# The first expert's weights fetched and split within the last feed-forward group

## The reference

```python
    logits = x @ w_gate
    e_idx = np.argmax(logits, axis=1)
    probs = softmax(logits); gate_w = probs[np.arange(N), e_idx]
    eom = 1.0 / (1.0 + np.exp(-(x @ w_output_gate)))
    for e in range(E):
        mask = e_idx == e
        h = np.maximum(x[mask] @ w1[e], 0.0)          # 512 -> 1024
        ye = h @ w2[e]                                # 1024 -> 512
        out[mask] = gate_w[mask, None] * eom[mask, e, None] * ye
```

## Time and profile before

| | us |
|---|---|
| runs of the kernel | 1080.41, 1082.92, 1083.64 (median 1082.92) |
| profiled execution | 1083.53, of which the span is 1081.2 |
| PE busy in the span | 1051.2 (97%) |
| DVE, ACT, POOL busy | 411.1, 293.1, 123.2 |

### The profile page before, as it was taken

One profiled execution on the slowest core, in us unless ns is written; L12 is line 12 of the kernel. 1 busy time (PEld: TensorE's weight loads), 2 busy tenths in 40 slices (PEclk: granted clock), 3 DMA queues, 4 the chain that ended last, 5 costly groups with the idle time before them and its releaser, 6 DMA issues.

```text
span 1081.2 us, 18273 instructions
## 1 busy us (share of the span) xinstructions
PE 1051.2 (97%) x6499; PEld 939.7 (87%) x6500; DVE 411.1 (38%) x794; ACT 293.1 (27%) x550; POOL 123.2 (11%) x113
## 2 busy tenths in 40 slices
PE   6989999999999999999999999998999999999997
PEld 5888999999999999999999999976788888888886
DVE  3454432323223223223222322458446444364542
ACT  2544332112112122121121121131334333243431
POOL 4770000000000000000000000023111211112111
PEclk9999999999999999999999999996999999999999
DMA  9996701001001001010010000060553533335311
GB/s 363 367 328 198 211 1 60 1 1 59 1 1 59 1 25 35 1 56 3 1 59 1 1 30 1 1 205 10 205 191 117 204 121 116 113 117 204 118 34 35
DMA packets 34090, 98.69 MB, mean 91 GB/s; under 512 B 4397, under 2 KB 10797, under 8 KB 34032
## 3 DMA queue, kind: packets, MB, share of 16 engines
q1 hardware_dynamic: 28976, 83.17, 22.5%
q0 software_dynamic: 4480, 13.90, 3.7%
q10 hardware_dynamic: 576, 0.79, 0.2%
HBM read 80.54 MB, written 18.09 MB: 91 GB/s over the span
## 4 chain that ended last, share of the span: by engine, by line
PE 93%; DMA 3%; DVE 3%; issue 0%; ACT 0%; POOL 0%; ACTq 0%; POOLq 0%; DVEq 0%
PE bank L941 37%; PE bank L959 18%; PE bank L1325 14%; PE bank L1301 13%; PE bank L1309 2%; PE bank L578 2%; DMA rows<-in_steps 2%; PE bank L529 1%; PE bank L630 1%; PE bank L543 1%; PE bank L564 1%; DMA qdec_t<-in_consts 1%; PE bank L744 1%; PE bank L753 1%; PE bank L1020 0%
## 5 line engine op out<-in xcount | busy, mean ns | idle before, releaser
L941 PE MATMUL bank<-x_hi,wab_hi 128*128 128x384 f32 x768 | 258.2, 336 | 0.0
L941 PE MATMUL bank<-x_hi,wab_lo 128*128 128x384 f32 x768 | 257.8, 336 | 0.0
L941 PE MATMUL bank<-x_lo,wab_hi 128*128 128x384 f32 x768 | 257.2, 335 | 0.0
L887 DVE TENSOR_TENSOR g_sb<-bank,b_sb 128x384 f32<-128x384 f32 x96 | 53.5, 557 | 370.9 <-PE bank L941 370.9
L941 PEld LDWEIGHTS bank<-x_hi,wab_hi 128*128 128x128 f32 x768 | 144.2, 188 | 4.2 <-issue 0.6
L941 PEld LDWEIGHTS bank<-x_lo,wab_hi 128*128 128x128 f32 x768 | 144.2, 188 | 3.6
L941 PEld LDWEIGHTS bank<-x_hi,wab_lo 128*128 128x128 f32 x768 | 144.1, 188 | 0.0
L705 ACT COPY b_sb<-bank 128x384 f32<-128x384 f32 x96 | 46.3, 482 | 257.3 <-PE bank L941 257.3
L959 PE MATMUL bank<-wo_hi,g_hi 128*128 128x512 f32 x288 | 115.7, 402 | 0.0
L959 PE MATMUL bank<-wo_hi,g_lo 128*128 128x512 f32 x288 | 113.4, 394 | 0.0
L959 PE MATMUL bank<-wo_lo,g_hi 128*128 128x512 f32 x288 | 113.2, 393 | 0.0
(11 more groups left out here) (161 smaller groups left out, 1201.0 us busy)
## 6 DMA issues: line engine op xcount, KB each, us to landing
raw<-in_w SPq DMA_DIRECT2D x64, 512.0 KB, 6.7
rows<-in_steps SPq DMA_DIRECT2D x20, 768.0 KB, 7.5
rows<-in_steps SPq DMA_DIRECT2D x24, 256.0 KB, 6.6
wab_raw<-in_weights SPq DMA_DIRECT2D x24, 256.0 KB, 7.2
x_dram<-y_sb SPq DMA_DIRECT2D x8, 768.0 KB, 4.1
xT_dram<-x_all SPq DMA_DIRECT2D x6, 768.0 KB, 12.1
x_raw<-xT_dram SPq DMA_DIRECT2D x6, 768.0 KB, 5.2
wo_raw<-in_weights SPq DMA_DIRECT2D x4, 768.0 KB, 9.7
```

The costliest lines, as they stand in the source:

```text
L887: nc.vector.tensor_tensor(g_sb[:, f % 2], bank[2 * (f % 2)][:, 0:GT], b_sb[:, f % 2], ALU.mult).then_inc(g_done, 1)
L941: ins = nc.tensor.matmul(bank[to][:, 0:GT], wab(w, f, j), x[s][:, k, :], start=(k == 0 and m == 0), stop=(k == KD - 1 and m == 2))
```

## The change

- **SP** loads w1 of expert 0 in the last group, two parts after step f=1 and two after f=3, and w2 likewise after f=5 and f=7, as the feed-forward weights under them fall free.
- **ACT** casts w1 after f=5 and f=6, three parts of w2 after the last step and the fourth behind the copies of y. **DVE** subtracts w1 after f=8, 9 and 10, and all of w2 in `dve_route`. **POOL** subtracts nothing any more.
- So that w1's two halves fit beside what is still in use, w1_hi and w1_lo share one buffer.
- **PE** transposes tile 1 into bank 3 directly behind the group, runs up(0) and puts the transposes of y and the logits between its matmuls; the last group's logits are made in strips as those of the other groups are (`pe_partial`, `pe_logits`). The sort stands within down(1), which is ahead of x_T(2) and up(2).
- POOL gathers tiles 2 and 3 together.

```diff
-    w1_hi = place("w1_hi", (P, 2 * KD * FE), F32R)
-    w1_lo = place("w1_lo", (P, 2 * KD * FE), F32R)
+    w1 = place("w1", (P, 2 * W1_SPAN), F32R)
+    w1_hi, w1_lo = w1[:, 0:W1_SPAN + KD * FE], w1[:, KD * FE:]
...
+    AT_W1_HI = {5: (0, 1), 6: (2, 3)}
+    AT_W1_LO = {AT_SCALE: (0, 1), AT_RANK: (2,), AT_FIRST: (3,)}
...
-                sp.wait_ge(a_done, GROUPS * KF)
-                load_expert(sp, raw1, w1_in, 0, raw1_in)
+                for half in range(2):
+                    sp.wait_ge(a_done, g * KF + 2 * half + 2)
+                    load_expert(sp, raw1, w1_in, 0, raw1_in, (2 * half, 2 * half + 1))
+                for half in range(2):
+                    sp.wait_ge(a_done, g * KF + 2 * half + 6)
+                    load_expert(sp, raw2, w2_in, 0, raw2_in, (2 * half, 2 * half + 1))
...
-        load_expert(sp, raw2, w2_in, 0, raw2_in)
...
+                if last and f in AT_W1_HI:
+                    split_w1(act, True, 0, AT_W1_HI[f])
...
-                split_w1(act, True, 0, (0,))
+                split_w2(act, True, 0, (0, 1, 2))
...
+                    if f in AT_W1_LO:
+                        split_w1(dve, False, 0, AT_W1_LO[f])
...
-        for t in range(TG):
-            pe.wait_ge(yT_read, TG * LAST + t + 1)
-            if t == 0:
-                pe.wait_ge(g_done, GROUPS * KF + 2)
-            for k in range(KD):
-                ins = nc.tensor.matmul(bank[3][:, t * 2 * NE:(t + 1) * 2 * NE], yT3[:, t, k, :], gates[:, k, :],
-                                       start=(k == 0), stop=(k == KD - 1))
-            ins.then_inc(logit_done, 1)
...
-        split_w1(dve, False, 0, (0,))
+        split_w2(dve, False, 0, (0, 1))
+        split_xe(dve, 1, 1)
...
-        split_w1(dve, False, 0, (1, 2))
-        dve.wait_ge(logit_done, TG * GROUPS)
-        v.tensor_copy(L3.rearrange("p t e -> p (t e)"), bank[3][:, 0:TG * 2 * NE]).then_inc(logit_read, TG)
+        split_w2(dve, False, 0, (2,))
+        dve_partial(dve, LAST, part_last)
+        split_w2(dve, False, 0, (3,))
+        dve_logits(dve, LAST)
...
-        split_xe(dve, 1, 1)
+        hT_rest(dve, 0)
...
-        hT_rest(dve, 0)
-
-        dve.wait_ge(w2_first_done, PARTS)
+        hT_rest(dve, 1)
...
-        split_w1(act, True, 0, (1, 2, 3))
+        split_w2(act, True, 0, (3,))
+        relu(0, True)
         act_exp(act, LAST)
         act_exp_og(act, LAST)
-        split_w2(act, True, 0, (0,))
-        relu(0, True, (0,))
-        split_w2(act, True, 0, (1,))
-        relu(0, True, (1,))
-        split_w2(act, True, 0, (2, 3))
...
-        part = slice((PARTS - 1) * PW, PARTS * PW)
-        pool.wait_ge(w1_hi_done, PARTS)
-        nc.gpsimd.tensor_tensor(w1_lo[:, part], raw1[:, part], w1_hi[:, part].bitcast(F32),
-                                ALU.subtract).then_inc(w1_first_done, 1)
-        for q in range(PARTS):
-            part = slice(q * PW, (q + 1) * PW)
-            pool.wait_ge(w2_hi_done, q + 1)
-            nc.gpsimd.tensor_tensor(w2_lo[:, part], raw2[:, part], w2_hi[:, part].bitcast(F32),
-                                    ALU.subtract).then_inc(w2_first_done, 1)
...
         gather(2)
+        gather(3)
...
-        pe_last_logits(pe)
-        up(0, 0, 0, {(0, 2): lambda: x_T(pe, 1, 1, 0, bank[4]), (1, 0): lambda: pe_counts(pe)})
-        pe.wait_ge(logit_read, TG * GROUPS + 1)
-        pe.wait_ge(h_read, 1)
-        up(1, 1, 0, {(1, 0): lambda: h_T(0)})
-        pe_sort(pe)
-        down(0, 0, None)
+        pe.wait_ge(g_done, GROUPS * KF + 2)
+        x_T(pe, 1, 1, 0, bank[3])
+        up(0, 0, 0, {(1, 0): lambda: pe_last_yT(pe), (1, 2): lambda: pe_partial(pe, LAST, yT_last)})
+        pe_logits(pe, LAST, part_last)
+        pe.wait_ge(h_read, 2)
+        up(1, 1, 0, {(1, 0): lambda: h_T(0), (1, 1): lambda: pe_counts(pe)})
+        down(0, 0, 0)
+        h_T(1)
+        down(1, 1, 0, {2: lambda: pe_sort(pe)})
         x_T(pe, 2, 0, 1, bank[4])
-        h_T(1)
...
         up(2, 0, run_of(run_even))
         x_T(pe, 3, 1, 1, bank[4])
-        down(1, 1, None)
         in_pairs(pe, pairs, pair)
```

More of the change, by code:

```diff
@@ L41 @@
 PW = KD * FE // PARTS
+W1_SPAN, W2_SPAN = 2 * KD * FE, KE * DM
 C_IDENT = 0
@@ L220, in build @@
     xe_lo = place("xe_lo", (P, 2, KD, P), F32R, where=x_raw_at + KD * GT * 4)
-    yT3 = place("yT3", (P, TG, KD, P), where=x_raw_at)
+    yT_last = place("yT_last", (P, KD, GT), where=x_raw_at)
     at[0] = x_raw_at
@@ L230, in build @@
     assert at[0] <= x_raw_at + KD * GT * 4
+    part_last = place("part_last", (P, GT), where=common)
     at[0] = common
@@ L634, in split_xe @@
         dve.wait_ge(xe_T_done, i + 1)
-        psum = bank[7 if isinstance(i, int) and i == 0 else 4].rearrange("p (k t) -> p k t", k=KD)
+        at_bank = {0: 7, 1: 3}.get(i, 4) if isinstance(i, int) else 4
+        psum = bank[at_bank].rearrange("p (k t) -> p k t", k=KD)
         nc.vector.tensor_copy(xe_hi[:, s], psum).then_inc(xe_done, 1)
@@ L638, in split_xe, with split_weight @@
         nc.vector.tensor_tensor(xe_lo[:, s], psum, xe_hi[:, s].bitcast(F32), ALU.subtract).then_inc(xe_done, 1)
-    def split_weight(eng, hi, run, raw, raw_in, w_hi_, w_lo_, hi_done, lo_done, parts):
+    def split_weight(eng, hi, run, raw, raw_in, w_hi_, w_lo_, span, hi_done, lo_done, parts):
         for q in parts:
-            to = bass.ds((run % 2) * (PARTS * PW) + q * PW, PW)
+            to = bass.ds((run % 2) * span + q * PW, PW)
             frm = raw[:, q * PW:(q + 1) * PW]
@@ L652, in split_w1 @@
     def split_w1(eng, hi, run, parts=range(PARTS)):
-        split_weight(eng, hi, run, raw1, raw1_in, w1_hi, w1_lo, w1_hi_done, w1_lo_done, parts)
+        split_weight(eng, hi, run, raw1, raw1_in, w1_hi, w1_lo, W1_SPAN, w1_hi_done, w1_lo_done, parts)
     def split_w2(eng, hi, run, parts=range(PARTS)):
-        split_weight(eng, hi, run, raw2, raw2_in, w2_hi, w2_lo, w2_hi_done, w2_lo_done, parts)
+        split_weight(eng, hi, run, raw2, raw2_in, w2_hi, w2_lo, W2_SPAN, w2_hi_done, w2_lo_done, parts)
     def in_groups(eng, group):
@@ L664, in in_groups, with load_expert @@
         group(GROUPS - 1, 1, False, True)
-    def load_expert(sp, raw, src, e, into):
-        for q in range(PARTS):
+    def load_expert(sp, raw, src, e, into, parts=range(PARTS)):
+        for q in parts:
             sp.dma_start(raw[:, q * PW:(q + 1) * PW],
@@ L745, in pe_yT, with pe_partial @@
         ins.then_inc(yT_done, 1)
-    def pe_partial(pe, g):
+    def pe_partial(pe, g, yT=yT_sb):
         pe.wait_ge(yT_read, TG * (g + 1))
@@ L752, in pe_partial, with pe_logits @@
             strip = slice(k * (P // KD), (k + 1) * (P // KD))
-            ins = nc.tensor.matmul(bank[7][strip, 0:GT], gates_pad[:, k, :], yT_sb[:, k, :], start=True, stop=True)
+            ins = nc.tensor.matmul(bank[7][strip, 0:GT], gates_pad[:, k, :], yT[:, k, :], start=True, stop=True)
         ins.then_inc(part_done, 1)
-    def pe_logits(pe, g):
+    def pe_logits(pe, g, part=part_sb):
         pe.wait_ge(part_read, g + 1)
         for t in range(TG):
-            ins = nc.tensor.matmul(bank[7][:, t * 2 * NE:(t + 1) * 2 * NE], part_sb[:, t * P:(t + 1) * P], sel, start=True, stop=True)
+            ins = nc.tensor.matmul(bank[7][:, t * 2 * NE:(t + 1) * 2 * NE], part[:, t * P:(t + 1) * P], sel, start=True, stop=True)
         ins.then_inc(logit_done, TG)
@@ L764, in dve_yT, with dve_partial @@
         nc.vector.tensor_copy(yT_sb[:, :, t * P:(t + 1) * P], bank[7].rearrange("p (k t) -> p k t", k=KD)).then_inc(yT_read, 1)
-    def dve_partial(dve, g):
+    def dve_partial(dve, g, part=part_sb):
         dve.wait_ge(part_done, g + 1)
-        nc.vector.tensor_copy(part_sb, bank[7][:, 0:GT]).then_inc(part_read, 1)
+        nc.vector.tensor_copy(part, bank[7][:, 0:GT]).then_inc(part_read, 1)
     def dve_logits(dve, g):
@@ L992, in build, with pe_last_yT @@
     LINKED = LAST * LINKS
-    def pe_last_logits(pe):
+    def pe_last_yT(pe):
         for t in range(TG):
@@ L1034, in dve_route @@
         link, count = linker(dve, LINKED)
-        split_w1(dve, False, 0, (0,))
+        split_w2(dve, False, 0, (0, 1))
+        split_xe(dve, 1, 1)
         for t in range(TG):
             dve.wait_ge(yT_done, TG * LAST + t + 1)
-            v.tensor_copy(yT3[:, t].rearrange("p k t -> p (k t)"), bank[4 + t]).then_inc(yT_read, 1)
-        split_w1(dve, False, 0, (1, 2))
-        dve.wait_ge(logit_done, TG * GROUPS)
-        v.tensor_copy(L3.rearrange("p t e -> p (t e)"), bank[3][:, 0:TG * 2 * NE]).then_inc(logit_read, TG)
+            v.tensor_copy(yT_last[:, :, t * P:(t + 1) * P], bank[4 + t].rearrange("p (k t) -> p k t", k=KD)).then_inc(yT_read, 1)
+        split_w2(dve, False, 0, (2,))
+        dve_partial(dve, LAST, part_last)
+        split_w2(dve, False, 0, (3,))
+        dve_logits(dve, LAST)
         dve_choose(dve, LAST, link)
@@ L1088, in dve_route @@
         link(v.tensor_copy(pair_i, e_end[:, NE - 1:NE]))
[L1089 to L1090 removed]
```

(15 more changed lines are left out.)

6 lines of the change are left out of this document (2 added, 4 removed).

## The result

Five runs of the changed kernel had a median of 1071.2 us (1068.1 to 1074.0), against 1080.4 us (1079.4 to 1083.6) for the kernel before on the same chip: a ratio of 0.9905, with a 95% interval of 0.9884 to 0.9925. The forecast was 1071.5 us.

A forecast was written before the change was run, and what follows sets the result against it. The prediction took PE waiting for DVE's routing chain at the handover from last group to experts as the bound. Gain 13.1 less 1.65 for clock, 11.45, from 1083.53 gives 1072.1; less 0.6 for the median, 1071.5 us; range 1068 to 1077.5.

The forecast's parts named there:

- PE's schedule: PE from the last group's end to up(3): step-by-step times, up(3) 13.1 us earlier before the clock's loss.
- DVE's slow rows: Routing chain on DVE: five instructions take about 2.1 us instead of 0.17 beside POOL's subtractions, about 9.8 us in all.
- Rival 3: DVE's slow instructions are not POOL's doing and stay; gain shrinks to 2.0, 1080.9 us; chance 0.05.
- The spare on DVE: Routing chain on DVE: tile_hot done at 740.1, PE wants it for the sort at 743.2, 3 us to spare.
- The gather: POOL's gather behind the sort: 4.98 us to landing, mostly covered by three quarters of down(1), 4.18.
- Rival 5: POOL's gather is held up by DVE, 2 us a time: 1073.5 us; chance 0.05.
- The clock: PE in the handover: one half-clock stretch, from waits for gather and xe(2) close together, costs 1.65 us.
- Rival 1: PE's clock stays up throughout the handover: 1069.8 us; chance 0.18.
- Rival 2: Clock falls at the wait before down(1), sort at half clock, and again after x_T(2): 1074.2 us; chance 0.22.
- The group's cover: Last feed-forward group: loads, casts and subtractions moved there fit in ACT's and DVE's idle time, costing nothing.
- Rival 4: ACT and DVE stretch the last group; slower than before, about 1090 us at 4.7 a piece; chance 0.04.
- The second expert's weights: First load 8.0 us after the sort's end, landing within 12.1; up to 2.7 late for ACT, costing nothing.

The follow-up runs named there:

- number 4: Changed kernel with two of the four w2 subtractions back on POOL, beside DVE's routing chain; one run, 1074.0 us.
- number 7: Changed kernel with all four w2 subtractions on POOL, each as soon as its cast is there, mostly ahead of the routing chain; one run, 1071.3 us.
- number 5: Changed kernel with five more unread 128x1024 subtractions on DVE, behind the first hT_lo and ahead of the counts; one run, 1079.6 us.
- number 6: Changed kernel with two more unread 128x1024 subtractions on DVE, behind the first hT_lo and ahead of the counts; one run, 1072.7 us.
- number 8: Changed kernel with each of the four w1 casts within the last group done three times on ACT; one run, 1067.7 us.
- number 3: Changed kernel with only the sort moved, between h_T(1) and down(1) instead of after a quarter of down(1); one run, 1065.8 us.
- number 2: Changed kernel with sort ahead of down(1), x_T(2) ahead of down(1)'s last eighth, x_T(3) inside up(2); four runs, 1066.8 us, 0.9840 of the kernel before.
- Number 1: Changed kernel with its early weights and strips of logits, but the old order on PE; four runs, 1069.1 us, ratio 0.9861 to the kernel before.

## Why the prediction was right, step by step

- **PE's schedule.** Predicted and measured from g: up(1) 8.87 and 9.13; down(0) 16.1 and 16.3; h_T(1) 21.7 and 21.75; down(1) 24.0 and 23.75; sort 25.4 and 25.3; x_T(2) 33.1 and 33.2; up(2) 35.5 and 35.6; up(3) with the one stretch at half clock 45.1 and 45.1. The y copies and those of yT stayed hidden. The largest miss of a single term is the step from h_T(1) to down(1), 2.00 instead of 2.33; most of it is made up by the step from the sort to x_T(2), which is 0.25 longer than predicted.
- **DVE's slow rows.** That they came from POOL was read off a coincidence in time; number 4 brought two of them back with two subtractions, and number 7 narrowed the cause. (The prediction has PE wait for DVE each time; two shorter waits of that stretch were 0.97 for ACT's copy of y and 0.24 for POOL's w_lo.) The held rows that the earlier trace rows show are tensor_tensor with both operands in SBUF (g and L, g and g, e and e); the other two of the five, in DVE's timeline of the kernel before, are casts from SBUF:

```profile
731.13 2.32 DVE L1045 CAST scale<-t_scale 128x24 fp32r<-128x24 f32 x1
...
735.31 2.23 DVE L1052 CAST e<-ei 128x8 f32<-128x8 int32 x1
```

The rows of number 7 that take an operand from a bank were not held. Rival 3 is out. The Trainium skill (SBUF — State Buffer, Who interferes with whom) has a rule for this: a DVE instruction with two SBUF inputs contends with a GpSimd instruction that reads SBUF, and so does a copy or cast in a two-port mode; one with at most one SBUF input outside these modes does not. Numbers 4 (2.28 and 2.24 instead of 0.18) and 7 (no row longer than in the changed kernel) agree with it; whether the two casts ran in such a mode no run here shows.
- **The spare on DVE.** This step failed: the prediction gave DVE's chain 3 us to spare. tile_hot came 22.4 after g (predicted 22.3), 2.9 ahead of the sort. But hT_lo(1) is queued behind tile_hot on DVE, and PE wants it for down(1), ahead of the sort. DVE's true spare was the 0.65 it stood waiting for hT_hi(1). It cost nothing here because nothing was late, which was luck and not foresight; numbers 4 to 6 show what it would have cost.
- **The gather.** The sort's start to x_T(2) is 752.39 - 744.47 = 7.92, of which 4.98 + 2.69 = 7.67 was predicted. The gather landed 3.5 after its issue, with the casts of the tile table beside it, against 3.4. Rival 5 is out.
- **The clock.** The count of one stretch was right. Its reason, waits close together, fits number 3, but number 2 had two such waits, one of them only 0.32, and no stretch; so what size they must have, and whether the wait before down(1) counts too, stays open. Rival 1 is out, since the stretch came. Rival 2 is out, since 0.96 before down(1) brought none. Length alone does not sort the waits: 2.72 in number 6 brought a stretch, 2.29 in number 4 did not, and 1.79 in the kernel before did.
- **The group's cover.** Cost nothing, as forecast. Rival 4's price, and the sentence that each us over comes on PE, were wrong: by its formula, casts of 3 x 0.98 would have cost at least 5.6 on ACT alone, and number 8 measured 0. The idle time of ACT was only a lower bound of the room.
- **The second expert's weights.** Issued 8.0 after the sort's end, at 755.27, as predicted; the first eight landed 9.7 after issue in the median, against 11.4, though the slowest took 13.0 and not 12.1. up(4) did not wait.
- **What the sum did not say.** It credited the 13.1 to feed and order together. Number 1 shows that the order alone is worth about -2.0 with this feed. This is the part of the mechanism that the prediction had wrong: it counted the new order as a gain. Number 3 shows that 4.0 come back by placing the sort where PE would otherwise wait, 2.4 of it by the start of up(2) and 1.6 as clock.
- **The size.** The medians differ by 9.2 us (8.1 to 12.5 by the interval of the ratio) and the traces by 11.4 at the handover, as forecast; g scatters over 5.5 us, which covers the difference. That the median lies 0.3 from the forecast is partly luck: the forecast counted from a median of 1082.92, and the same 11.4 taken from the 1080.4 of the five runs would have given 1069.0.

## What to carry to other kernels

When one engine's small instructions are slow now and then, look at what another engine reads in just those microseconds, and move that work beside instructions of another kind; here the feed that did so paid without the new order of matmuls, and the order did not add to it. The spare of a chain is measured to the first consumer of anything queued behind it on its engine, not to the consumer of its own result. Idle time before an eviction bounds the room for extra work from below only; doubling or tripling that work shows in one run whether there is more.

## What the runs showed of the hardware

A stretch at half clock also came where PE had not waited. Behind 21 matmuls of only two columns (the sort that forms the two known tiles, 2.48 us), four of the ten profiled executions ran on at half clock (numbers 1, 2, 3 and 5). In number 2:

```profile
704.29 2.48 PE L881 MATMUL bank<-hot_first,off_hot 128*128 128x2 f32 x21
...
708.20 0.63 PE L970 MATMUL bank<-wo_hi,g_hi 128*128 128x512 f32 x1
```

The other six, with the same instructions there, did not. What decides it stays open.
